# The row blocks of one second-layer slot matrix, loaded behind the last dispatch instead of beside the fourth batch of scores

## The reference

```python
logits = x @ phi                       # 3072 x 32
d = softmax(logits, axis=0)            # over the tokens
slot_input = d.T @ x                   # 32 x 384, "dispatch"
for e in range(8):
    h = relu(slot_input[4e:4e+4] @ w1[e])     # 384 x 1024, first layer
    slot_out[4e:4e+4] = h @ w2[e]             # 1024 x 384, second layer
c = softmax(logits, axis=1)            # over the slots
out = c @ slot_out                     # "combine"
```

## Time and profile before

| what | value |
|---|---|
| time of three runs | 380.25, 381.19 and 381.48 us, median 381.19 us |
| the profiled execution | span 387.5 us from its first to its last instruction, mean granted PE clock 0.969 |
| PE busy | 354.1 us, 91% |
| DVE, ACT, POOL busy | 281.8, 221.0 and 115.0 us |
| DMA | 97.58 MB, 252 GB/s over the span |

### The profile page before, as it was taken

How to read it: one execution, slowest core, us unless ns; L and a number is a source line. 1 busy time by engine, 2 the same in 40 slices (tenths; PEclk the granted TensorE clock), 3 DMA queues, 4 the chain that set the end, 5 groups by cost and what they waited for, 6 DMA issues and landing times.

```text
span 387.5 us, 14814 instructions
## 1 busy us (share of the span) xinstructions
PE 354.1 (91%) x5880; PEld 269.6 (70%) x5880; DVE 281.8 (73%) x564; ACT 221.0 (57%) x681; POOL 115.0 (30%) x179
## 2 busy tenths in 40 slices
PE   6699999999999999889999999999999999679990
PEld 6487777877777788656777777777777777345360
DVE  7999999999999634786676767777677776430371
ACT  3777888778887755134656556565555664200060
POOL 3543322343223340254222233332221224540000
PEclk9989999999999999989999999999999999689996
DMA  8987656766568995013193799495858779759438
GB/s 310 415 305 265 241 198 216 257 258 248 197 205 286 424 402 205 3 23 111 29 393 128 300 323 393 178 361 193 325 211 321 263 259 396 281 170 327 167 152 336
DMA packets 31300, 97.58 MB, mean 252 GB/s; under 512 B 4062, under 2 KB 14410, under 8 KB 29722
## 3 DMA queue, kind: packets, MB, share of 16 engines
q1 hardware_dynamic: 29466, 93.81, 65.2%
q0 software_dynamic: 1792, 3.17, 2.7%
HBM read 85.53 MB, written 11.45 MB: 250 GB/s over the span
## 4 chain that ended last, share of the span: by engine, by line
PE 56%; DVE 5%; another core or an unknown queue 3%; issue 1%; POOL 1%; ACT 1%; DVEq 0%; ACTq 0%
PE a_bank L772 19%; PE y_bank L781 18%; PE y_bank L928 3%; PE a_bank L944 3%; PE a_bank L637 2%; DVE x_all L1550 2%; PE sums_bank L705 1%; PE a_bank L832 1%; PE y_bank L598 1%; PE y_bank L593 1%; PE ktok_bank L645 1%; PE sums_bank L645 1%; PE y_bank L605 1%; PE y_bank L740 0%
## 5 line engine op out<-in xcount | busy, mean ns | idle before, releaser
L781 PE MATMUL y_bank<-w_sb,work 128*32 128x192 f32 x1664 | 78.5, 326 | 0.5 <-ACT work L1131 0.5
L772 PE MATMUL a_bank<-w_sb,work 128*32 128x256 f32 x1248 | 77.9, 382 | 0.1
L781 PEld LDWEIGHTS y_bank<-w_sb,work 128*32 128x32 f32 x1664 | 64.9, 110 | 8.8 <-DVE work L1396 1.1
L1586 POOL TENSOR_SCALAR_AFFINE_SELECT a_sb<-a_sb 128x512 f32<-128x512 f32 x48 | 44.2, 932 | 86.7 <-ACT a_sb L1016 86.7
L772 PEld LDWEIGHTS a_bank<-w_sb,work 128*32 128x32 f32 x1248 | 42.4, 109 | 25.6 <-issue 13.0
L1026 ACT ACTIVATE bonus_v<-v_sb,bonus 128x48 f32<-128x48 f32 x192 | 45.0, 321 | 14.0 <-DVE x_all L1260 13.9
L1104 ACT ACTIVATE work<-work 32x96 f32<-32x96 f32 x108 | 30.4, 281 | 39.3 <-PE a_bank L772 37.0
L1440 DVE TENSOR_TENSOR ys<-work 32x192 f32<-32x192 f32 x104 | 37.0, 355 | 9.9 <-ACT work L1131 9.2
L1396 DVE STREAM_TRANSPOSE work<-hid 128x256 f32<-128x256 f32 x53 | 23.6, 446 | 26.2 <-PE y_bank L781 22.9
L572 PE MATMUL a_bank<-r_in,k_in 64*128 64x128 f32 x384 | 31.0, 295 | 0.1
L572 PEld LDWEIGHTS a_bank<-r_in,k_in 64*128 64x128 f32 x384 | 24.7, 193 | 6.3 <-issue 5.7
(11 more groups left out here) (314 smaller groups left out, 582.6 us busy)
## 6 DMA issues: line engine op xcount, KB each, us to landing
w_sb<-in_moe_w SPq DMA_DIRECT2D x20, 1536.0 KB, 11.7
wrk_sb<-in_wrk SPq DMA_DIRECT2D x16, 768.0 KB, 7.0
e_sb<-in_moe_w SPq DMA_DIRECT2D x8, 1536.0 KB, 11.0
wrk_sb<-in_wrk SPq DMA_DIRECT2D x15, 780.0 KB
v_sb<-in_vt SPq DMA_DIRECT2D x16, 288.0 KB, 2.9
tokens<-x_all SPq DMA_DIRECT2D x4, 1152.0 KB, 21.7
out<-x_all SPq DMA_DIRECT2D x12, 384.0 KB, 3.9
x_all<-in_moe_w SPq DMA_DIRECT2D x2, 1536.0 KB
```

The lines of the kernel that those rows point to most:

```text
L772: last = nc.tensor.matmul(out[SUB * g:SUB * (g + 1), 0:FB], x[:, kk, :], w1_sb[j][:, kk, FB * g:FB * (g + 1)], start=(kk == 0), stop=(kk = ...
L781: last = nc.tensor.matmul(bank[4][SUB * g:SUB * (g + 1), 0:YW], h_t[:, SUB * k:SUB * (k + 1)], w2_sb[j][:, k, d:d + YW], start=(b == 0), s ...
L1586: nc.gpsimd.affine_select(out=x, in_=x, compare_op=ALU.is_gt, fill=0.0, base=0, pattern=[[0, 2], [0, 2], [1, C]], channel_multiplier=-1).t ...
```

## The change

Three things are edited. On SP the three DMAs of `e2[4]` are taken from behind `stage_ready` and put behind `slot_parts_full` 3, and `e1[7]`, which waits for `slot_parts_full` 2, now comes first. On PE the wait for `ld_e1[1]` moves from group 13 to group 16 (groups 13 to 15 are no longer overwritten before the dispatch), and the wait for `ld_e2[0]` at group 26 is gone. On POOL the awaited number is 32 instead of 48 with 13 groups or fewer: one matrix, `e1[5]`, has to have landed, not also the blocks.

```diff
             load_e1(sp, 5)
             sp.wait_ge(ld_e2[0], 16)
-            sp.wait_ge(stage_ready, 1)
+            sp.wait_ge(slot_parts_full, 2)
+            load_e1(sp, 7)
+            sp.wait_ge(slot_parts_full, 3)
             load_e2_blocks(sp, 0, 3, ld_e1[5 % EH])
             load_e2_blocks(sp, 3, 7, ld_e2[0])
             load_e2_blocks(sp, 7, 8, ld_e2[0])
-            sp.wait_ge(slot_parts_full, 2)
-            load_e1(sp, 7)
-            sp.wait_ge(slot_parts_full, 3)
             sp.wait_ge(ld_e2[5 % EH], 16)
...
-            last_landed = pe.value_load(tiles_i[0:1, E + 5:E + 6], min_val=16, max_val=48)
+            last_landed = pe.value_load(tiles_i[0:1, E + 5:E + 6], min_val=16, max_val=32)
...
             dispatch(3 * BATCH, LAST_GROUPS, B1, MAX_GROUPS, x_sorted, bank[1])
+            dispatch(LAST_GROUPS, 4 * BATCH, B1, MAX_GROUPS, x_sorted, bank[1])
             pe.wait_ge(ld_e1[5 % EH], last_landed)
-            dispatch(LAST_GROUPS, 4 * BATCH, B1, MAX_GROUPS, x_sorted, bank[1])
             pe.wait_ge(disp_ready, 5)
             dispatch(4 * BATCH, MAX_GROUPS - 2, B1, MAX_GROUPS, x_sorted, bank[1])
-            pe.wait_ge(ld_e2[0], last_landed)
             dispatch(MAX_GROUPS - 2, MAX_GROUPS, B1, MAX_GROUPS, x_sorted, bank[1])
...
-            nc.gpsimd.tensor_scalar(tiles_i[:, E + 5:E + 6], batches_up[:, 2:3], -16.0, 48.0, ALU.mult, ALU.add).then_inc(counts_ready, 1)
+            nc.gpsimd.tensor_scalar(tiles_i[:, E + 5:E + 6], batches_up[:, 2:3], -8.0, 32.0, ALU.mult, ALU.add).then_inc(counts_ready, 1)
```

## The result

The changed kernel takes 383.21 us (median of 6 runs, 383.05 to 383.96), the kernel before on the same chip 380.4 us (6 runs, 379.25 to 381.48). The ratio is 1.0075, with a 95% interval of 1.0048 to 1.0103: about 2.8 us slower. The forecast was 378.4 us; the time lies in the range, the direction was wrong.

A forecast was written before the change was run, and what follows sets the result against it. PE's work bounds the kernel, plus two tail holds where its signals arrive late beside small-packet loads. Terms: -3.1 - 1.6 + 1.8 + 0.1 = -2.8 us, 387.5 to 384.7 profiled; with runs 6.3 us below, 378.4 us, range 375.5 to 383.6.

The forecast's parts named there:

- The holds: In the profiled tail, PE's signals reach other engines late: 3.45 us at the fourth scores, 2.1 us behind the last dispatch.
- The landings: Loads behind the last dispatch run in one line; combine weights slip about 0.5 us under 1.37 us of cover: 0.
- The first hold: At the fourth scores, with the blocks gone, DVE's L1484 starts on time and PE's L887 moves from 333.44 to 330.38: -3.1 us.
- PE's clock: Without the idle gap at the fourth scores, PE keeps full clock where 0.50 was granted from 333.4 to 339.3: -1.6 us.
- The second hold: Behind the last dispatch, 1.57 MB more rows lengthen PE's late signals, +1.8 us; the lower clock behind may last longer, +0.1.
- Waits taken from PE: In PE's dispatch, moving one wait and dropping one gives 0, since both loads had already landed.
- the number on POOL: POOL's changed awaited number is the same instruction and costs nothing.
- `e1[7]`: On SP's queue, this load is issued no later than 332.19 and no longer behind the blocks: 0.
- The holds belong to the profiled execution: Rival: the late signals are absent or covered in the runs, so nothing moves: 0 to -0.5, 381.1 us; chance 0.17.
- The hold moves: Rival: the path clogs wherever the rows are put, so the lateness shifts behind the last dispatch: +0.4, 381.6 us; chance 0.18.
- the loop of L870: Rival's cause: PE leaving its late-batch loop makes the fourth-scores lateness, which stays; only the one at L914 grows; chance 0.19.
- The slower side: Case: lateness at ACT's L1176 grows with the moved blocks, +4.1 us, 385.3 us; chance 0.19, outcome slower 0.23.

The follow-up runs named there:

- no blocks (9): Changed kernel without any load of `e2[4]`, its product left out of the output, on chip C: 379.07 us, ratio 0.9969 to the kernel before.
- three moved (3): Changed kernel with only the three blocks over groups 13 to 15 moved behind the last dispatch, five left at `stage_ready`: 379.98 us, ratio 0.9976 to before.
- four less (2): Changed kernel without the load of the middle four blocks of `e2[4]` (0.79 MB less): 380.04 us, ratio 0.9985 to the kernel before.
- before (1): The unchanged kernel profiled a second time: 381.36 us, span 379.6 us.
- nine idle products (12): Changed kernel with nine idle products on PE ahead of its wait for the combine weights, on chip D: 382.58 us, ratio 1.0053 to before.
- after (8): The changed kernel run again, unaltered, on chip C: 383.47 us, ratio 1.008 to the kernel before.
- experiment 11: Kernel before with PE's two loops over late batches (L870, L914) written out straight: 380.19 us, ratio 0.9983 to before.
- experiment 4: Changed kernel with `e2[7]` issued behind the four loads of combine weights instead of ahead: 383.41 us, ratio 1.0061 to before.

## Where the prediction was right or wrong

Two steps of the prediction failed. The holds and the clock behind them were carried from the profiled execution into the runs, net -2.8 us; in the runs they are about 0. And "The landings" were put at 0, where the runs show 2.4 to 3.0 us of loss: the line of loads behind the last dispatch had about 2.5 us of slack for the 4.1 us that were added to it. The first took the forecast gain away, the second made the kernel slower.

Two lengths, read from the PE rows, put the runs in one order: from the first slot product (L928 before, L926 after) to the turns of the combine weights, and from there to the end of the span.

| kernel | MB behind the last dispatch for `e2[4]` | to the turns, us | turns to end, us | median, us |
|---|---|---|---|---|
| no blocks (9) | 0 | 359.31 − 337.47 = 21.8 | 377.3 − 359.31 = 18.0 | 379.07 |
| three moved (3) | 0.59 | 359.03 − 337.13 = 21.9 | 377.5 − 359.03 = 18.5 | 379.98 |
| four less (2) | 0.79 | 360.89 − 338.64 = 22.3 | 379.1 − 360.89 = 18.2 | 380.04 |
| before (1) | 0, moved at the scores | 361.13 − 338.06 = 23.1 | 379.6 − 361.13 = 18.5 | 380.3 |
| nine idle products (12) | 1.57 | 362.53 − 337.90 = 24.6 | 381.0 − 362.53 = 18.5 | 382.58 |
| after | 1.57 | 361.82 − 337.44 = 24.4 | 381.4 − 361.82 = 19.6 | 383.21 |
| after (8) | 1.57 | 362.46 − 337.76 = 24.7 | 382.3 − 362.46 = 19.8 | 383.47 |

After less before: 1.3 to 1.6 us in the first length (the line), 1.1 to 1.4 in the second (the clock), together 2.4 to 3.0, where the runs differ by 2.8 and 3.35. The trace of experiment 11, which has the loads as before, gives 23.0 and 18.5 us, as the row "before". By medians the nine idle products split it a little otherwise, 0.6 to 0.9 for the clock and about 2.3 (382.58 less 380.31) for the rest; some 0.7 us of that rest I can't place in a row.

**The first hold, "-3.1", and PE's clock behind it, "-1.6".** Wrong for the runs. Against the execution that was profiled first the sizes are about right (by PE's rows, -3.1 from the scores to L887 and -2.2 from there to L909), but the blocks are not what made the difference, for the second profile has neither the hold nor the low clock with the blocks in place. Both terms should have been about 0. The prediction had the warning in its own text, "That the runs are shorter by about the size of both holds with their clock", and carried the 6.3 us over unchanged. This step accounts for the gain that did not come; the loss comes from "The landings" below.

**The second hold, "+1.8" and "+0.1".** Wrong in the same way, and in direction even against the first profile: from PE's L909 to the first slot product it is 345.60 − 342.02 = 3.6 us there and 337.44 − 336.29 = 1.15 in the changed kernel, 2.4 less, with 1.57 MB more of rows behind the dispatch. No unknown piece stands there; ACT's L1174 starts at 337.14, 0.1 us behind the end of PE's L907 (336.29 + 0.75), which released it.

**The landings, "They slip by about 0.5 us ... 1.37 us of cover, so 0".** This is the step that made the kernel slower. The mechanism was named, the size was off. The line was laid from 342.6 us, a start delayed by the second hold, and its end before (358.5) was taken as the end of expert loads, where the second profile has the loads of expert weights end at 350.5, some 2.5 us of nearly idle DMA engines, and then the combine weights. And the cover of 1.37 us was PE's lateness from the holds: in the second profile there is none, PE waits 1.17 us for the weights already before the change. The sentence "That cover is gone if the chain ahead gets shorter by more than that against the line of transfers; the last 0.5 us then shows" held, except that 1.3 us showed by the trace and about 2 by the medians, and that the wait took PE's clock with it, which no term had.

**What nothing in the sum had.** All eight blocks at the fourth scores slow POOL's chain of scatters; the change frees it (the last scatter is issued 2.4 us earlier) and so might have gained up to 1.0 us (experiment 9), had the line not been full.

**Waits taken from PE, the number on POOL, `e1[7]`: "0".** Right. No idle time stands in PE's dispatch rows.

**The rivals.** "The holds belong to the profiled execution" (0.17) was right on the holds and wrong in its price, because it had no term for the line. "The hold moves" and the loop of L870 as the place of a loss are refuted for chips A, C and D: no hold, both loops present. On B the loop is not refuted. The slower side came, by none of the mechanisms priced: its 385.3 rested on a growing hold, and the true one was the line in "The landings". A rival built from that part, the line with no holds, would have been the one to have: 1.57 MB or 4.1 us added to a line whose slack was about 2.5 us.

## What to carry to other kernels

Compare the profiled execution with the runs before a row of it is believed: where it is 6 us longer, the rows that make it so belong to it, and the cover that they give to others is not there in the runs. When loads are moved to a later place, lay the whole line on the shared DMA engines up to the next consumer and count its idle stretches: here the first 0.8 MB left the kernel at the time of before (1.0 us over the kernel without any), and the next 0.8 MB cost 3.2 us. A load may be cut to fit that slack, and swapping order or queue mainly chooses which consumer waits; a wait of PE of 2.5 us was followed by a slower stretch here and one of 1.5 us was not, so a longer wait should be priced with what may follow it.

## What the hardware showed that I had not expected

- On one of four chips the kernel before takes 388.0 us instead of 380.1 to 380.4. Three changed kernels profiled there show DVE idle for 5.7 and 3.0 us at the fourth scores while PE's work is recorded as done, with the DMA engines at 0.07, and a shorter lateness of 1.1 to 1.7 us behind the last dispatch. The first profile of before is late at the fourth scores and behind the last dispatch too. What it is stays open.
- Behind waits of PE of 2.48, 2.79 and 3.64 us the granted clock was 0.52 (361.8 to 365.2 us), 0.63 (362.4 to 366.0, experiment 8) and 0.58 (362 to 366, experiment 4); behind waits of 1.54, 1.17 and 0.53 us it stayed at 1.00.
- An idle product of 128x128 in fp32 is two matmul instructions and 0.24 us (4.73 us for 20 at full clock).
